# A fused attention, soft-MoE and MLP kernel on one core: the beginning laid out anew, identity transposes in TensorE's gaps, and the second-stage weights loaded in another order

## The reference

```python
# 1: gated linear attention, B, H, S, D = 4, 8, 768, 48
f = 1.0 / (1.0 + np.exp(-f_logit))
for t in range(S):
    state = f[:, :, t, :, None] * state + np.einsum('bhd,bhe->bhde', k[:, :, t], v[:, :, t])
    y[:, :, t] = np.einsum('bhd,bhde->bhe', q[:, :, t], state)
# 2: soft MoE on x = y as (3072, 384), phi 384 x 32, 8 experts, w1 384 x 1024, w2 1024 x 384
logits = x @ phi
d = softmax of logits over the tokens;  slot_input = d.T @ x
slot_out[e] = np.maximum(slot_input[e] @ w1[e], 0.0) @ w2[e]
x = (softmax of logits over the slots) @ slot_out
# 3: MLP, w_in 384 x 2048, w_out 2048 x 384
h = x @ w_in
out = (h - np.tanh(h)) @ w_out
```

## Time and profile before

| | us |
|---|---|
| median of 3 runs | 536.1 |
| lowest and highest of them | 534.45, 542.52 |
| profiled execution, its own time | 535.02 |
| its span, first to last instruction | 533.3 |
| PE busy | 491.3 (92%) |
| PEld busy | 433.2 (81%) |
| DVE busy | 390.3 (73%) |
| ACT busy | 232.2 (44%) |

### The profile page before, as it was taken

How to read it: one execution, slowest core, us unless ns; L and a number is a source line. 1 busy time by engine, 2 the same in 40 slices (tenths; PEclk the granted TensorE clock), 3 DMA queues, 4 the chain that set the end, 5 groups by cost and what they waited for, 6 DMA issues and landing times.

```text
span 533.3 us, 19169 instructions
## 1 busy us (share of the span) xinstructions
PE 491.3 (92%) x8171; PEld 433.2 (81%) x8171; DVE 390.3 (73%) x571; ACT 232.2 (44%) x436; POOL 101.0 (19%) x183
## 2 busy tenths in 40 slices
PE   4779989899989989899997899999999999999997
PEld 3668878788878878877733499999999999999997
DVE  3578878888888888753461599977777777777773
ACT  3146656666665656535330464322322322323222
POOL 6244434444444444400020000000000000000000
PEclk9989999999999999869998999999999999999999
DMA  6766666666676755161799700100100100100101
GB/s 111 127 138 138 146 151 142 147 138 152 150 155 136 162 121 135 40 219 42 257 373 397 277 1 1 61 0 0 59 0 0 59 0 0 59 0 6 53 1 59
DMA packets 122231, 56.17 MB, mean 105 GB/s; under 512 B 102320, under 2 KB 115632, under 8 KB 121776
## 3 DMA queue, kind: packets, MB, share of 16 engines
q1 hardware_dynamic: 122160, 55.11, 39.6%
HBM read 50.38 MB, written 4.72 MB: 103 GB/s over the span
## 4 chain that ended last, share of the span: by engine, by line
PE 77%; ACT 7%; issue 7%; DVE 5%; DMA 3%; DVEq 0%; ACTq 0%
PE far_ps L934 9%; PE far_ps L926 9%; PE far_ps L930 9%; PE turn_ps L553 6%; PE far_ps L620 6%; PE out_ps L704 5%; PE near_ps L582 4%; PE out_ps L934 3%; ACT scores L1041 3%; PE out_ps L930 3%; PE out_ps L926 3%; DMA w_late<-in_moe_w 3%; DVE state L1311 3%; PE turn_ps L662 2%; PE turn_ps L913 2%
## 5 line engine op out<-in xcount | busy, mean ns | idle before, releaser
L926 PE MATMUL far_ps<-w_out_hi,g_hi 128*128 128x384 f32 x288 | 83.7, 341 | 0.3
L934 PE MATMUL far_ps<-w_out_hi,g_lo 128*128 128x384 f32 x288 | 82.4, 337 | 0.0
L930 PE MATMUL far_ps<-w_out_lo,g_hi 128*128 128x384 f32 x288 | 82.0, 335 | 0.0
L1518 DVE TENSOR_TENSOR g_lo<-g,g_hi 128x512 fp32r<-128x512 f32 x96 | 66.4, 692 | 3.0
L1158 ACT ACTIVATE tanh_h<-turn_ps 128x512 f32<-128x512 f32 x48 | 28.7, 599 | 75.2 <-PE turn_ps L913 75.1
L1158 ACT ACTIVATE tanh_h<-near_ps 128x512 f32<-128x512 f32 x48 | 28.8, 599 | 69.1 <-PE near_ps L913 68.6
L934 PEld LDWEIGHTS far_ps<-w_out_hi,g_lo 128*128 128x128 f32 x288 | 54.4, 189 | 3.7
L1041 ACT ACTIVATE scores<-far_ps 16x192 f32<-16x192 f32 (+2 forms) x124 | 49.6, 401 | 13.7 <-PE far_ps L620 12.0
L553 PE MATMUL turn_ps<-ident,raw 128*112 128x128 f32 x288 | 46.2, 301 | 9.6 <-DVE one L1323 5.9
L926 PEld LDWEIGHTS far_ps<-w_out_hi,g_hi 128*128 128x128 f32 x288 | 53.0, 188 | 1.9 <-ACT out_rows L1164 1.6
L930 PEld LDWEIGHTS far_ps<-w_out_lo,g_hi 128*128 128x128 f32 x288 | 52.7, 188 | 0.5 <-DVE w_out_lo L1482 0.2
(11 more groups left out here) (170 smaller groups left out, 888.3 us busy)
## 6 DMA issues: line engine op xcount, KB each, us to landing
w_sb<-in_moe_w SPq DMA_DIRECT2D x48, 256.0 KB, 3.8
w_xt<-in_moe_w SPq DMA_DIRECT2D x4, 1536.0 KB, 9.7
raw<-in_q SPq DMA_DIRECT2D x32, 144.0 KB, 3.0
raw<-in_k SPq DMA_DIRECT2D x32, 144.0 KB, 3.2
raw<-in_f_logit SPq DMA_DIRECT2D x32, 144.0 KB, 3.9
vt<-in_v SPq DMA_DIRECT2D x32, 144.0 KB, 3.7
out_rows_dram<-out_rows SPq DMA_DIRECT2D x24, 192.0 KB, 1.9
w_rows<-in_moe_w SPq DMA_DIRECT2D x2, 1536.0 KB, 15.9
```

The lines of the kernel that those rows point to most:

```text
L926: pe.matmul(o_banks[t][:, 0:DM], g_hi[ft % 4][:, t * P:(t + 1) * P], w_out_hi[:, ft, :], start=(ft == 0), stop=False)
L930: pe.matmul(o_banks[t][:, 0:DM], g_hi[ft % 4][:, t * P:(t + 1) * P], w_out_lo[:, ft, :], start=False, stop=False)
L934: return pe.matmul(o_banks[t][:, 0:DM], g_lo[ft % 4][:, t * P:(t + 1) * P], w_out_hi[:, ft, :], start=False, stop=(ft == FT - 1))
L1518: dve.tensor_tensor(g_lo[ft % 4][:, :], g[ft % 2][:, :], g_hi[ft % 4][:, :].bitcast(F32), ALU.subtract).then_inc(parts_done, 1)
```

## The change

It has six parts.

1. **Beginning, loads.** SP no longer loads unit 0's gates (f); ACT does, on its own queue, after one small sigmoid on `one`, which makes the sigmoid's table the first that ACT loads. The memset of `one` comes first on DVE, and PE waits for `pads_made` 2 instead of 3, that is for `one` and the pads of `raw`, and no longer for the memsets of scores, out_ps and far_ps. Those count a new semaphore, `cleared`, for which their first users wait.
2. **Beginning, PSUM.** Unit 0's keys are turned into near_ps instead of turn_ps, so that `turn_keys(0)` waits only for k; `turn_gates(0)` waits for the copy of the queries.
3. **Identity turned in the gaps.** `keep_clock(times)` transposes the identity into an unused part of PSUM: 12 times ahead of everything, 12 times ahead of `level_2(0)`, 6 times ahead of `level_3(0)`, 8 times ahead of `level_2(1)`. Its results are read by nobody.
4. **POOL.** Masks 3 and 4 are made behind the first unit's `pair_products` and `quad_products`.
5. **Phi round.** `logits_round(0)` moves from behind `within(A, 0)` to the place right behind `level_4(Z)` (A and Z are the last two units).
6. **Weights.** `w2_early` is loaded in eight pieces of 192 KB, each behind a wait of its own. The third part of `x_tok` moves to batch 1's place in `xt`, so that `load_w2(0, 1)` goes to batch 0's place and waits for 6 turned tiles instead of 12. `w2_late` has its own semaphore, and SP issues w_in only when the other three w2 tiles of round 1 have landed.

The following rows show where instructions stand. First PE's first instructions, before: the transposes of queries, keys and gates (L553), level 1 (L582), the next queries and level 2 (L607).

The diff, without the declarations of semaphores and with its context cut:

```diff
--- before.py
+++ after.py
@@ -139,7 +139,7 @@
...
     THIRD = B * NC // 3
-    rows_at = [top[0], early_end, region_c]
+    rows_at = [top[0], early_end, region_c + size([P, HC * DM])]
     x_tok = [at(f"x_tok{i}", [P, THIRD, DM], F32, rows_at[i]) for i in range(3)]
@@ -152,8 +152,8 @@
...
     w2_late = at("w2_late", [P, HC * DM], F32, softmax_at)
-    w2_at = [[w2_early[:, :], w2_xt[:, 1, :], w2_xt[:, 2, :], w2_xt[:, 3, :]],
-             [w2_xt[:, 0, :], w2_rows[0][:, :], w2_rows[1][:, :], w2_late[:, :]]]
+    w2_at = [[w2_early[:, :], w2_xt[:, 0, :], w2_xt[:, 2, :], w2_xt[:, 3, :]],
+             [w2_xt[:, 1, :], w2_rows[0][:, :], w2_rows[1][:, :], w2_late[:, :]]]
@@ -358,7 +365,8 @@
...
                 sp.dma_start(w2_at[r][j].rearrange("p (k n) -> p k n", k=HC),
-                             w2[EG * r + j].rearrange("(k p) n -> p k n", p=P)).then_inc(w2_loaded[r], 16)
+                             w2[EG * r + j].rearrange("(k p) n -> p k n", p=P)
+                             ).then_inc(late_loaded if (r, j) == (1, EG - 1) else w2_loaded[r], 16)
@@ -379,10 +387,10 @@
...
-            for x in (2, 1, 0):
+            for x in (2, 1):
                 load_rows(0, x)
             turn_loads(-1, [])
-            sp.wait_ge(pads_made, 2)
+            sp.wait_ge(pads_made, 3)
             for h in range(H):
@@ -395,21 +403,40 @@
...
             load_w1([early])
+            def load_early(k):
+                sp.dma_start(w2_early[:, k * DM:(k + 1) * DM], w2[0][k * P:(k + 1) * P, :]).then_inc(early_loaded, 16)
             sp.wait_ge(scored[3], UNITS)
...
             sp.wait_ge(y_done[1], UNITS - 2)
-            load_w2(0, 0)
+            load_early(0)
             sp.wait_ge(scored[4], UNITS)
             load_w1([early + 2])
+            sp.wait_ge(own_done, UNITS - 1)
+            load_early(1)
+            sp.wait_ge(within_done, 2 * (UNITS - 2) + 1)
+            load_early(2)
             sp.wait_ge(far_scored, UNITS)
             load_w1([early + 3])
+            sp.wait_ge(y_done[0], UNITS - 1)
+            load_early(3)
+            sp.wait_ge(ends_turned, UNITS)
+            load_early(4)
             sp.wait_ge(within_done, 2 * (UNITS - 1))
-            load_w1([early + 4, early + 5])
+            load_w1([early + 4])
+            sp.wait_ge(own_done, UNITS)
+            load_early(5)
+            load_w1([early + 5])
+            sp.wait_ge(y_done[1], UNITS - 1)
+            load_early(6)
+            sp.wait_ge(within_done, 2 * UNITS)
+            load_early(7)
...
             for j in range(1, EG):
-                sp.wait_ge(x_turned, (j + 1) * NC)
+                sp.wait_ge(x_turned, (1, 3, 4)[j - 1] * NC)
                 load_w2(0, j)
@@ -419,6 +446,7 @@
...
             sp.wait_ge(hidden_done, 1)
+            sp.wait_ge(w2_loaded[1], 16 * (EG - 1))
             for kc in range(KC):
@@ -442,11 +470,12 @@
...
             pool.memset(decay[:, :, 0:1], 0.0).then_inc(consts_made, 1)
-            made = 0
-            pool.wait_ge(consts_made, CONSTS)
-            for x, (nb, h, step, keys) in enumerate(((HALF, 1, 2, 1), (HALF, 1, 2, 2), (16, 2, 4, 2), (8, 4, 8, 4),
-                                                     (4, 8, 16, 8))):
+            MASK_FORMS = ((HALF, 1, 2, 1), (HALF, 1, 2, 2), (16, 2, 4, 2), (8, 4, 8, 4), (4, 8, 16, 8))
+            def make_mask(x):
+                nb, h, step, keys = MASK_FORMS[x]
+                made = x * MASK_STEPS
                 for i in range(2):
@@ -523,8 +551,17 @@
...
+            pool.wait_ge(consts_made, CONSTS)
+            make_mask(0)
+            make_mask(1)
+            make_mask(2)
+            pair_products(0)
+            quad_products(0)
+            make_mask(3)
+            make_mask(4)
             for n in range(UNITS):
-                if there(n):
+                if 0 < n:
                     pair_products(n)
@@ -547,16 +584,19 @@
...
         def _(pe):
-            def turn(n, x):
+            def turn(n, x, bank=turn_ps):
...
                 for c in range(NC):
-                    mm = pe.transpose(turn_ps[0:R, c * P:(c + 1) * P],
+                    mm = pe.transpose(bank[0:R, c * P:(c + 1) * P],
                                       raw[:, x, c, :, :].rearrange("p h d -> p (h d)")[:, 0:R], ident[:, :])
...
                 pe.wait_ge(f_loaded, n * 32 + 32)
-                pe.wait_ge(keys_kept, n + 1)
+                if n:
+                    pe.wait_ge(keys_kept, n + 1)
+                else:
+                    pe.wait_ge(queries_kept, 1)
                 turn(n, 0).then_inc(gates_turned, 1)
@@ -569,8 +609,9 @@
...
                 pe.wait_ge(k_loaded, n * 32 + 32)
-                pe.wait_ge(queries_kept, n + 1)
-                turn(n, 1).then_inc(keys_turned, 1)
+                if n:
+                    pe.wait_ge(queries_kept, n + 1)
+                turn(n, 1, keys_ps(n)).then_inc(keys_turned, 1)
@@ -627,6 +668,8 @@
...
                     pe.wait_ge(far_merged, n)
+                else:
+                    pe.wait_ge(cleared, RING + 2)
@@ -730,7 +773,13 @@
...
             pe.wait_ge(consts_made, 2)
-            pe.wait_ge(pads_made, 3)
+            def keep_clock(times, place=far_ps[:, 0:P]):
+                for x in range(times):
+                    pe.transpose(place, ident[:, :], ident[:, :])
+            keep_clock(12)
+            pe.wait_ge(pads_made, 2)
             for n in range(-1, UNITS):
@@ -743,6 +792,10 @@
...
                     turn_queries(n + 1)
+                if n == 0:
+                    keep_clock(12)
+                if n == 1:
+                    keep_clock(8, out_ps[:, NC * BK:NC * BK + P])
                 if there(n):
@@ -753,6 +806,8 @@
...
                     within(n - 2, 1)
+                if n == 0:
+                    keep_clock(6)
                 if there(n):
@@ -764,11 +819,11 @@
...
             level_4(Z)
-            block_states(A)
-            within(A, 0)
             pe.wait_ge(consts_loaded, 16 * H)
...
             logits_round(0)
+            block_states(A)
+            within(A, 0)
             far_level(Z)
@@ -843,7 +898,11 @@
...
                     pe.wait_ge(hidden_t_ready, r + 1)
-                    pe.wait_ge(w2_loaded[r], 16 * EG)
+                    pe.wait_ge(w2_loaded[r], 16 * (EG - 1))
+                    if r == 0:
+                        pe.wait_ge(early_loaded, 16 * HC)
+                    else:
+                        pe.wait_ge(late_loaded, 16)
                 for hc in range(x * HC // 2, (x + 1) * HC // 2):
@@ -995,7 +1054,7 @@
...
                     act.wait_ge(ends_turned, n - RING + 1)
-                act.activation(qk[n % RING][0:R, 2, :], turn_ps[0:R, 0:S], ACT.Copy).then_inc(keys_kept, 1)
+                act.activation(qk[n % RING][0:R, 2, :], keys_ps(n)[0:R, 0:S], ACT.Copy).then_inc(keys_kept, 1)
@@ -1057,6 +1116,11 @@
...
                     act.activation(dst, src, ACT.Copy).then_inc(x_read[0], 1)
+            act.wait_ge(pads_made, 1)
+            act.activation(small[0:1, 8:9], one[0:1, 0:1], ACT.Sigmoid)
+            for h in range(2):
+                act.dma_start(raw[:, 0, :, h, 0:D], by_head[0][:, h, :, :]).then_inc(f_loaded, 16)
@@ -1265,6 +1330,8 @@
...
                         dve.wait_ge(within_done, 2 * (n - RING + 1))
+                    else:
+                        dve.wait_ge(cleared, n + 1)
                 if n == 0:
@@ -1317,10 +1384,9 @@
...
             for s in scores:
-                dve.memset(s[:], 0.0)
-            dve.memset(out_ps[:], 0.0)
-            dve.memset(far_ps[:, 512:1536], 0.0)
-            dve.memset(one[:], 1.0).then_inc(pads_made, 1)
+                dve.memset(s[:], 0.0).then_inc(cleared, 1)
+            dve.memset(out_ps[:], 0.0).then_inc(cleared, 1)
+            dve.memset(far_ps[:, 512:1536], 0.0).then_inc(cleared, 1)
             dve.wait_ge(consts_made, CONSTS)
```

7 lines of the change are left out of this document (6 added, 1 removed).

## The result

The changed kernel takes **530.7 us** (median of 20 runs, 524.93 to 542.34) against 539.24 for the kernel before (20 runs beside it): ratio 0.9865, 95% interval [0.9833, 0.9897]. All ratios here leave out the slow runs of either kernel, those more than 1.5% above its fastest, so that they differ from the quotient of the medians. Timed again in two later series it gave 0.9824 [0.9748, 0.99] (e14, 6 runs) and 0.9941 [0.9902, 0.998] (e18, 12 runs). The range (518.5 to 531.0) just reaches that. Of the three chances the one for within 2% (0.45) came true and not the larger one for faster (0.53).

What follows compares the result with a forecast made beforehand. The prediction took PE as the bound, with 77% of the chain of waits. From 535.6 us it subtracted 6.8 (beginning), 0 (phi round) and 4.4 (weights), 11.2 together, giving 524.4 us; range 518.5 to 531.

Steps and rivals of the forecast that it cites:

- The base: Starting time for the whole kernel before: 535.6 us, the middle of three timed runs and the profiled execution.
- The beginning, 6.8: First units: earlier level 1 and full clock sooner bring the third unit's start 6.8 us forward.
- issued behind the table load: Unit 0's loads: gates issued on ACT's queue after its table load; keys then land at 6.7, queries still at 4.6.
- Then the low stretch at 30.8 goes too: Before the third unit: low clock from 30.8 vanishes, transposes and far level shorten, 1.5 us less before ACT's merge.
- The middle, unchanged: Units after the third: ACT and DVE pass them on as before, everything merely shifting by the beginning's 6.8 us.
- The fourth rival: Middle units: the clock falls more often and the kernel gets slower, 537.9 with three more falls; chance 0.04.
- The phi round and the weights' pieces, 0: Last units: moving the phi round costs nothing (bounds 0.8 saved, 1.0 lost); w2_early's eight pieces change nothing.
- The weights, 4.4: Experts: PE's 2.8 us wait for w2_late and 1.6 us of low clock vanish, so `first_slots` starts 4.4 us earlier.
- w_in overtakes w2_late: Expert loads: 0.9 MB of w_in went ahead of w2_late, costing 2.4 us; the new wait recovers 1.6 to 2.4.
- the wait goes entirely: Experts: w2_late lands at 285.3 to 286.1, before PE needs it at 286.54, removing the 2.82 us wait.
- The 1.6 us for the low clock behind the wait: Experts, 289.36 to 294.25: low clock behind PE's wait for w2_late also goes, saving 1.6 us.
- The third rival: Experts: the weights bring nothing, w2_late staying relatively late or w_in replacing its wait; 528.3 us, chance 0.12.

Runs made afterwards that it cites:

- e14: The changed kernel, unchanged, run and profiled again; 532.57 us, ratio 0.9824.
- e18: The changed kernel, unchanged, timed beside the kernel with the early w2 tile in one transfer; 533.95 us, ratio 0.9941.
- e2: The changed kernel with unit 0's gates (f) loaded by SP behind the keys, as before the change; 531.42 us, ratio 0.9843.
- e13: The kernel before, unchanged, run again for a second profile; 540.21 us.
- e16: The kernel before, unchanged, run again for a third profile; 544.92 us.
- e12: The changed kernel with the early w2 tile in one transfer at the place of its first piece; 537.87 us, ratio 0.9936.
- e17: The changed kernel with the early w2 tile in one transfer, timed beside the unedited changed kernel; 535.14 us, ratio 0.9947.
- e5: The changed kernel without SP's new wait ahead of w_in; 531.31 us, ratio 0.9909.
- e6: The changed kernel with SP's wait ahead of w_in extended until w2_late too has landed; 537.55 us, ratio 0.9997.
- e4: The changed kernel with the phi round and the weights as before, so the beginning alone; 536.26 us, ratio 0.9943.
- e3: The kernel before with the weight part alone (eight pieces, tile order, w_in's new wait); 537.86 us, ratio 0.9965.
- e9: The kernel before with the phi round's move alone; 540.36 us, ratio 0.9928.

## Why the size was wrong

The direction was right; the sum was too large and stood on too low a base. Of the 6.3 us between forecast and measurement 3.6 are the base and 2.7 the terms. The steps that failed are the two named below under the beginning and the weights.

**The base.** 535.6 came from three runs and a profile; 20 runs have a median of 539.24, and the 137 runs of before in all series 539.5. What it hid: I argued the middle units "as before", from a profile in which they had no low clock.

**The beginning, 6.8.** Measured 5.6 in the profile pair, 4.9 on the means of three (37.25, 32.36), 4.6 over all profiles with either beginning (five, nine). The step that failed is "issued behind the table load": ACT's DMA issue stands at 0.98, inside the table load (0.81 to 2.09), so f shares the engines with q, whose second transfer I had at 4.6 and which came at 5.9. The 0.8 us lost there are still there at every landmark: level 1 at 10.46 for 9.7, level 2 at 15.00 for 14.2, that of unit 1 at 25.57 for 24.7. e2 gives 0.85 back. "Then the low stretch at 30.8 goes too" also failed in after, where it moved to 32.0 and tripled; in e14 and e18 it went.

**The middle, unchanged.** So it is on the mean (183.3 and 182.8), but with 0.39 us for each us of low clock and 0 to 31 of them it decides what a single run shows. The fourth rival (the clock falls more often) was right that falls of the middle units can eat the gain, and wrong in taking the change for their cause: before has them too.

**The phi round and the weights' pieces, 0.** The stretch from the sixteenth sigmoid to the sums over tokens shrank from 47.4 to 44.1 (means of three). The fall 7 to 8 us behind the sixteenth sigmoid is in one of three on either side and so is not the difference; where it is missing, before has 47.3 and 47.4 and after 43.1 and 42.9, and e13 and e16 have the stall with its fall. e12 and e17 tie that stall to the whole tile. The gain came from a line that I costed at nothing: the pieces "issued between about 228 and 244 and read at 280: nothing". A transfer that is early enough for its reader can still be in the way of PE's own work.

**The weights, 4.4.** Measured 1.2 to 1.6 (three profiles of before 35.9 with a fall in one, three of after 34.3). The step that failed is that w_in overtakes w2_late ("2.4 us") and that the new wait takes this back: it was worth nothing (e5, e6), and so "the wait goes entirely" failed too: 1.3 to 1.9 us of it stay in every profile with the new order. The 1.6 us for the low clock behind the wait were counted on a fall that two of before's three profiles do not have. The third rival (the weights bring nothing) was nearer.

**The sum.** 4.9 + 0.5 + 3.2 + 1.6 = 10.2, by three profiles against three. That this is so near to 11.2 is luck: a term put at nothing brought 3.2 and hid that the two others were 4.7 too large together. The timed runs say 6.7. After's three profiles have 16.2 us of low clock on the mean and its 38 timed runs 24.5, before's 29.8 and, on 117 timed runs, 32.2: at 0.26 us each this flatters the profiles' difference by 1.5; the other 2 stay open. The parts alone, by their ratios times 540: the beginning 3.1 (e4, interval 0.5 to 5.6), the weights 1.9 (e3, -0.5 to 4.3), the phi round 3.9 (e9, -0.4 to 8.2): too wide to settle the terms one by one, which only the stretches of the table do. Open too is why the clock falls 7 to 8 us behind the sixteenth sigmoid in some runs and not in others.

## What to carry to other kernels

Take more than one profile, and more than three runs, before costing a stretch as "unchanged": if its clock can fall, its time is a distribution. Do not read a single row as the rule either: six transposes at full clock in one profile of the changed kernel were at half speed in its two others. A large transfer well ahead of its reader isn't free; look at what else uses the DMA engines then, an engine's instructions among it. Filling an idle TensorE with transposes brought landmarks forward where it waits anyway, and won nothing where it is the bound.

## What the runs showed of the hardware

**PE stands still in step with its instruction queue.** Over all 20 profiles PE stood still between the third and the sixteenth sigmoid 257 times for over 0.45 us with nothing to wait for that the profile shows. 248 of these stalls end 1.2 to 1.7 us behind the end of a 16 KB packet of the instruction queue (median 1.43), where packets come every 4.3 to 4.7 us on the median; a moment picked at random lies there with a chance of 0.11. So PE seems to run out of instructions and to go on when the next ones have come.

**Such stalls precede falls of the clock.** Of the 59 falls between the third sigmoid and 26 us behind the sixteenth (20 profiles), 45 had a stall of 0.75 us or more end in the 4 us before; any stretch of that length at full clock has one with a chance of 0.13. Nine of the other 14 are the fall behind the sixteenth sigmoid. Of 82 stalls of 1 us or more at full clock, 42 were followed by a fall. No run took the stalls away, so that they cause the falls is argued and not shown, save that the whole tile brought both behind the sixteenth sigmoid, and in pieces it brought no stall over 1.14 us and no fall there.

**Low clock and time.** Over 292 runs, each compared with the mean of its own kernel and series, each us at the lower level costs 0.26 us (standard error 0.015), and 0.39 (0.05) in the middle stretch of 19 profiles.
